# First and third GEMM by Strassen's seven products, with first result and activations kept in fp32 and split where they are used

## The chip, the cores and the metric

The kernel runs on one core of one Trainium2 chip. The metric is the device time of one execution in microseconds (us), and less is better. Five engines work side by side, each through its own list of instructions in the order in which the program writes them, and meet only at semaphores: PE (TensorE, the matmuls), DVE (VectorE), ACT (ScalarE), POOL (GpSimd) and SP, which here only issues the DMAs.

## The reference, cut to what matters

```
x = attn(q, k, v, cap)            # 2 batches, 12 heads, 448 tokens, head size 64; scores go through cap*tanh(s/cap)
x = x as 896 tokens x 768
h = x @ w_in                      # 768 x 2048, the first GEMM
g = max(0.01 * h, h)
y = g @ w_out                     # 2048 x 768, the second GEMM
yn = y / sqrt(mean(y*y) + 1e-6) * rms_g
gate = yn @ w_gate                # 768 x 1536 each: together the third GEMM
val  = yn @ w_val
out = (gate * sigmoid(gate) * val) @ w_out2     # 1536 x 768, the fourth GEMM
```

All is fp32. The matmuls run on fp32r operands: each fp32 operand is split into a rounded part (`hi`) and what is left (`lo = x - hi`), and a product is made of three matmuls, `w_hi*x_hi`, `w_hi*x_lo` and `w_lo*x_hi`.

## The kernel before

All arrays are held transposed, features on the 128 partitions and tokens on the free axis, 448 tokens of one batch to a tile. Five stages follow each other on PE.

**Attention** goes through 12 pairs of heads. For each pair PE makes scores (L611, L615) and weighs the values (L629, L633); ACT does tanh and exp (L348, L354). DVE splits q and k (`split_qk`, L432, L434), takes the result out of PSUM (`keep_x`, L442), inverts the sums that came back through a DMA (L448, L452), multiplies (`normalise`, L459) and splits the pair's x tile (L462 for `x_hi`, L464 for `x_lo`). PE cannot weigh the next pair before `keep_x` of the last one.

**First GEMM** (`unit_in`, L647): 32 units, one for each of 16 feature tiles and each batch, of 6 contraction tiles times 3 matmuls. DVE makes `w_hi` (L472), POOL `w_lo` (L296), both double buffered. The result goes through `leak` on ACT (L360), `g_full` on DVE (L478), `g_hi` on ACT (L365) and `g_lo` on DVE (L483), so that all of g lies split in SBUF when it is used.

**Second GEMM** (`unit_out`, L673): 6 output tiles of two halves, 48 matmuls each, and both batches in turn on each weight tile. ACT squares (L386), POOL sums the squares (L309), DVE scales by `rms_g` (L535), ACT and DVE split the result (L390, L541). The work behind one output tile lies beside the matmuls of the next.

**Third GEMM** (`unit_gv`, L693): 24 units of 36 matmuls, a gate and a value unit for each of 12 tiles. The sum of squares (L703) and the spread of the reciprocal root (L711) sit between the first three units. DVE multiplies (L566, L569, L572, L579), ACT does the sigmoid (L406) and `act_hi` (L410), POOL `act_lo` (L321). The fourth GEMM's weights are split during the stage (L584 on DVE, L327 on POOL).

**Fourth GEMM** (L736): 14 groups of 36 matmuls with 384 columns; ACT takes them out (L424) and SP stores them.

The order on each engine is written by hand; no scheduler moves anything. SP issues the loads in the order in which they are used, each waiting for its buffer.

## Time and profile before

| what | value |
|---|---|
| median of 3 runs | 620.59 us (620.0 to 622.28) |
| the profiled execution's own time | 620.48 us |
| its span, first to last instruction | 618.7 us |
| DVE, ACT, POOL busy | 282.0, 161.3, 203.5 us |

The span is what the rows below cut up; 1.78 us of the execution's time lie outside it. Busy time of PE counts matmuls that overlap each other in the pipeline, so the step from one matmul to the next is read from the length of a stretch over its count of matmuls. A stall of PE is a gap between such stretches.

### The profile page before, as it was taken

Reading aid. Unit: us, or ns where it says so; the run is one execution under the profiler, and the core shown is the slowest. Engines: PE = TensorE matmul, PEld = TensorE weight load, DVE = VectorE, ACT = ScalarE, POOL = GpSimd, SP = SyncE. Lnnn points to the kernel's source line nnn. Section 1 sums busy time; section 2 is a strip of 40 time slices with the busy share of each in tenths; the row PEclk is TensorE's granted clock in tenths of the full one; section 3 lists DMA queues with packets and bytes.
Section 4 is the critical chain, followed back from the end, with each engine's and each line's share of the span. In section 5 each row is a group of like instructions: output and inputs, shape, how many; then the busy total and the mean of one; then the engine's idle time right before and its main releaser. Section 6 shows DMA issues by size and latency. Waiting matters only on the chain.

```text
span 618.7 us, 7411 instructions
## 1 busy us (share of the span) xinstructions
PE 601.8 (97%) x2988; PEld 527.3 (85%) x2988; DVE 282.0 (46%) x383; ACT 161.3 (26%) x227; POOL 203.5 (33%) x124
## 2 busy tenths in 40 slices
PE   4999999989999999999999999999999999999998
PEld 3556554779999999999999999999999999999997
DVE  3286664688788883332133226344545443110000
ACT  5777775122333220111011222111111111100000
POOL 1020000245455553343353425453545352332000
PEclk9999999999999999999999999999999999999999
DMA  6145542243333332121211211212212220123101
GB/s 208 33 108 125 124 125 46 77 131 105 105 120 107 102 120 91 46 69 34 69 39 47 77 52 51 77 52 77 70 58 77 57 71 2 51 59 121 38 26 38
DMA packets 31586, 47.75 MB, mean 77 GB/s; under 512 B 17216, under 2 KB 19008, under 8 KB 31552
## 3 DMA queue, kind: packets, MB, share of 16 engines
q1 hardware_dynamic: 31552, 47.29, 26.1%
q8 instruction: 23, 0.38, 0.2%
q14 instruction: 11, 0.09, 0.1%
...
## 4 chain that ended last, share of the span: by engine, by line
PE 90%; DVE 4%; DMA 2%; POOL 1%; ACT 1%; issue 1%; SPq 0%; DVEq 0%
PE ps L693 28%; PE ps L673 19%; PE ps L647 17%; PE ps L736 13%; PE ps L629 7%; PE ps L611 2%; PE ps L633 2%; DMA qk_raw<-in_qk 1%; PE ps L615 1%; DVE x_norm L459 1%; DMA sums<-x_raw 1%; DVE g_lo L483 1%; POOL w_lo L296 1%; DVE x_raw L442 1%; ACT probs L354 1%
## 5 line engine op out<-in xcount | busy, mean ns | idle before, releaser
L296 POOL TENSOR_TENSOR w_lo<-w_raw,w_hi 128x768 fp32r<-128x768 f32 (+1 forms) x68 | 132.6, 1950 | 323.8 <-DVE w_hi L472 323.8
L472 DVE CAST w_hi<-w_raw 128x768 fp32r<-128x768 f32 (+1 forms) x68 | 39.5, 582 | 187.5 <-issue 119.8
L693 PE MATMUL ps<-x_hi,w_hi 128*128 128x448 f32 x288 | 82.0, 366 | 0.0
L693 PE MATMUL ps<-x_lo,w_hi 128*128 128x448 f32 x288 | 81.8, 365 | 0.0
L693 PE MATMUL ps<-x_hi,w_lo 128*128 128x448 f32 x288 | 81.8, 365 | 0.0
L647 PE MATMUL ps<-x_hi,w_hi 128*128 128x448 f32 x192 | 70.5, 367 | 2.9 <-POOL w_lo L296 2.9
L647 PE MATMUL ps<-x_hi,w_lo 128*128 128x448 f32 x192 | 70.1, 365 | 0.0
L647 PE MATMUL ps<-x_lo,w_hi 128*128 128x448 f32 x192 | 70.1, 365 | 0.0
L483 DVE TENSOR_TENSOR g_lo<-g_full,g_hi 128x448 fp32r<-128x448 f32 x32 | 61.0, 1910 | 0.0
L629 PE MATMUL ps<-probs,v_ones 128*128 128x448 f32 x144 | 56.2, 540 | 2.1 <-DVE x_raw L442 2.1
L693 PEld LDWEIGHTS ps<-x_hi,w_lo 128*128 128x128 f32 x288 | 54.1, 188 | 4.3
L693 PEld LDWEIGHTS ps<-x_lo,w_hi 128*128 128x128 f32 x288 | 54.1, 188 | 4.3
L693 PEld LDWEIGHTS ps<-x_hi,w_hi 128*128 128x128 f32 x288 | 53.9, 188 | 4.3
L673 PE MATMUL ps<-g_lo,w_hi 128*128 128x448 f32 x192 | 54.7, 366 | 0.0
L673 PE MATMUL ps<-g_hi,w_lo 128*128 128x448 f32 x192 | 54.7, 366 | 0.0
L673 PE MATMUL ps<-g_hi,w_hi 128*128 128x448 f32 x192 | 54.7, 366 | 0.0
L629 PEld LDWEIGHTS ps<-probs,v_ones 128*128 128x128 f32 x144 | 27.1, 190 | 25.8 <-issue 25.4
L647 PEld LDWEIGHTS ps<-x_hi,w_hi 128*128 128x128 f32 x192 | 36.1, 188 | 7.5 <-POOL w_lo L296 4.1
L348 ACT ACTIVATE probs<-ps 128x896 f32<-128x896 f32 (+1 forms) x48 | 36.8, 816 | 21.6 <-PE ps L611 21.6
L673 PEld LDWEIGHTS ps<-g_hi,w_lo 128*128 128x128 f32 x192 | 36.1, 188 | 3.1
L673 PEld LDWEIGHTS ps<-g_hi,w_hi 128*128 128x128 f32 x192 | 36.0, 188 | 3.1
L673 PEld LDWEIGHTS ps<-g_lo,w_hi 128*128 128x128 f32 x192 | 36.1, 188 | 3.1
...
## 6 DMA issues: line engine op xcount, KB each, us to landing
w_raw<-in_w_in SPq DMA_DIRECT2D x32, 384.0 KB, 3.0
...
w_raw<-in_w_gate SPq DMA_DIRECT2D x12, 384.0 KB, 2.9
w_raw<-in_w_val SPq DMA_DIRECT2D x12, 384.0 KB, 3.0
v_raw<-in_w_out SPq DMA_DIRECT2D x12, 384.0 KB, 3.0
...
```

Of the source, the lines that this page charges most:

```text
L296: pool.tensor_tensor(w_lo[u % 2][:, 0:n], w_raw[u % 2][:, 0:n], w_hi[u % 2][:, 0:n].bitcast(F32), ALU.subtract).then_inc(w_lo_done, 1)
L348: act.activation(tiles(probs_of(p, i, n), S), ps[:, bank_of(p, i):bank_of(p, i) + n, 0:S], ACT.Tanh, scale=scale_reg).then_inc(tanh_done, 1)
L354: act.activation(c, c, ACT.Exp, scale=cap_reg, bias=capc[:, 6:7]).then_inc(exp_done, 1)
L472: dve.tensor_copy(w_hi[u % 2][:, 0:n], w_raw[u % 2][:, 0:n]).then_inc(w_hi_done, 1)
L483: dve.tensor_tensor(lo[:, cols(u % N1)], g_full[u % 2][:, :], hi[:, cols(u % N1)].bitcast(F32), ALU.subtract).then_inc(g_lo_done, 1)
L611: last = pe.matmul(ps[:, bank + h, 0:S], k[HEAD[h], k_c], q[HEAD[h], 0:S], start=(k is hi and q is hi), stop=(k is lo))
L629: pe.matmul(ps[:, PV + h, 0:S], v_ones[p % 2][:, c:c + 128], probs[p % 2][:, (2 * t + h) * S:(2 * t + h + 1) * S], start=(t == 0), stop=False)
L633: last = pe.matmul(ps[:, PV + h, 0:S], v_ones[p % 2][HEAD[h], c:c + 128], probs[p % 2][HEAD[h], 2 * MAIN * S:(2 * MAIN + 1) * S], start=Fa ...
L647: last = pe.matmul(ps[:, HP + u % 2, 0:S], w[u % 2][:, c * 128:(c + 1) * 128], x[:, (b * KD + c) * S:(b * KD + c + 1) * S], start=(c == 0 ...
L673: last = pe.matmul(ps[:, 2 * (m % 2) + b, 0:S], w[half][:, (f % HALF_F) * 128:(f % HALF_F + 1) * 128], g_parts[b][g][:, f * S:(f + 1) * S] ...
L693: last = pe.matmul(ps[:, 4 * fp + 2 * s + b, 0:S], w[s][:, c * 128:(c + 1) * 128], x[:, (b * KD + c) * S:(b * KD + c + 1) * S], start=(c = ...
L736: last = pe.matmul(ps[:, n % 8, 0:NHALF], a[:, c], w[half][:, f * NHALF:(f + 1) * NHALF], start=(f == 0 and a is act_hi and w is v2_hi), s ...
```

## The change

Strassen's scheme (in Winograd's form) multiplies two matrices cut in 2 by 2 blocks with seven block products in place of eight. Here the blocks are the two halves of the contraction (3 tiles of 128 each), two feature tiles (in the third GEMM the gate tile and the value tile) and the two batches. A unit, `s`, is seven products of 9 matmuls (`product`): 8 units are the first GEMM, 12 the third. Each product has its own combination of x blocks (B11, T1, T3, T2, B22, B21, T4) and of weight blocks.

- x combinations are made once, before each of the two GEMMs: 21 tiles are split in place of 12. `combine` makes them in the attention (DVE makes T1 to T4 and all `x_hi`, POOL all `x_lo`); `first_half`, `second_half`, `t2_t3`, `t4`, `y_hi`, `y_lo`, `y_lower` make them in the second GEMM and behind it (DVE, ACT and POOL).
- Weight combinations are made for each unit: four `s_part` on DVE, 384 wide. `w_hi` is moved from DVE to ACT (`weight_hi`), `w_lo` stays on POOL (`weight_lo`), now 384 wide (256 in the second GEMM), in a ring of seven instead of two.
- Results are put together from PSUM on DVE: `take_p5`, `take_p7`, `take_p6`, and four more additions for each unit. P3, P2 and P4 add into banks that hold an earlier product, so PE waits there for `a_done`, `p1_kept` and `a2_done`.
- g stays in fp32. `g_hi` (ACT) and `g_lo` (DVE) split two tiles for each of the 48 steps of the second GEMM, into a ring of two steps; the second GEMM is now 3 passes over all of g, two output tiles by two batches each (`unit_out`, 12 matmuls for a step).
- The activations stay in fp32 as well and are split for each of the 7 token tiles of the fourth GEMM (`split_act` on ACT, `split_lower` on DVE). Its weights are split in the last gate and value unit (`value_hi` on ACT, `value_lo` on DVE, L490 on POOL), four raw buffers deep.
- silu is one activation; the second factor of the norm is put into the output's scale, where L572 was a multiplication.

The core of the diff:

```diff
-            def unit_in(u):
-
-                b = u // N1
-                pe.wait_ge(w_lo_done, u + 1)
-                if u < 2:
-                    pe.wait_ge(tanh_done, T * PAIRS)
-                at_least(pe, g_done, u - 1)
-                pe.wait_ge(x_lo_done, (b + 1) * NP)
-                for c in range(KD):
...
+            def product(s, j, c_tiles=range(KH)):
+                n = widx(s, j)
+                if c_tiles[0] == 0:
+                    pe.wait_ge(w_lo_done, n + 1)
+                    bank_free(s, j)
+                for c in c_tiles:
+                    x_ready(s, j, c)
+                    w_c = slice(n % 7 * HALF + c * 128, n % 7 * HALF + (c + 1) * 128)
                     for w, x in ((w_hi, x_hi), (w_hi, x_lo), (w_lo, x_hi)):
...
+            def unit_out(i):
+
+                q, f = divmod(i, N1)
+                n = W_OUT + i
+                pe.wait_ge(w_lo_done, n + 1)
+                pe.wait_ge(g_lo_done, 2 * i + 2)
...
+            def g_hi(i):
+
+                f = i % N1
+                if i < N1:
+                    act.wait_ge(g_done, 4 * (f // 2 + 1))
+                if i > 1:
+                    act.wait_ge(prod_done, count[W_OUT + i - 2])
+                for b in range(B):
+                    act.activation(ring_hi[:, cols(2 * (i % 2) + b)], g_tile(2 * f + b), ACT.Copy).then_inc(g_hi_done, 1)
...
+            for i in range(STEPS):
+                q, f = divmod(i, N1)
+                weight_lo(W_OUT + 5 + i)
+                if q > 0 and f in (3, 7):
+                    m = 2 * (q - 1) + (f == 7)
+                    add_squares(m, 0)
+                    add_squares(m, 1)
+                if q > 0 and f in (4, 8):
+                    m = 2 * (q - 1) + (f == 8)
+                    if m < KH:
+                        y_lo(B11, m)
+                    else:
+                        y_lo(B22, 0)
+                        y_lo(B21, 0)
...
+            s = U1
+            pe.wait_ge(sq_done, 2 * (KD - 2))
+            pe.wait_ge(scaled_done, 2 * (KD - 2))
+            product(s, P1)
+            product(s, P5)
+            pe.wait_ge(sq_done, 2 * (KD - 2) + 1)
+            pe.wait_ge(scaled_done, 2 * (KD - 2) + 2)
+            product(s + 1, P1)
+            pe.wait_ge(sq_done, 2 * KD - 1)
+            pe.wait_ge(scaled_done, 2 * KD)
+            product(s + 1, P5)
             pe.wait_ge(acc_done, 2 * KD)
...
+            for c in range(KH):
+                for j in (P7, P6, P3, P2):
+                    product(s, j, range(c, c + 1))
+                if c == 1:
+                    pe.wait_ge(rinv_done, 1)
...
+            keep_p1(UNITS - 1)
+            for k in range(7):
+                value_hi(k)
+            silu(UNITS - 1, 1)
+            value_hi(7)
+            value_hi(8)
+            value_hi(9)
+            silu(UNITS - 1, 0)
+            split_act(0, *pieces_of(0)[0])
```

Three places show how the instructions stand. First DVE in the attention, one pair's turn near the end (`r_bc` holds the pair's normalised x, `sq_67` and `sq_68` its T1 and T2; line numbers are those of each kernel's own file). Before:

```order
L448 SCALAR_TENSOR_TENSOR sums_eps<-sums_61 128x7
L452 RECIPROCAL recip_64<-sums_eps 128x7
L459 TENSOR_TENSOR x_norm<-x_raw_86,recip_row_88 64x448 x2
L462 CAST x_hi<-x_norm 128x448
L464 TENSOR_TENSOR x_lo<-x_norm,x_hi 128x448
L442 COPY x_raw_86<-ps 65x896
```

Now, for pairs 6 to 8:

```order
L711 RECIPROCAL recip_76<-sums_eps 128x7
L719 TENSOR_TENSOR r_bc<-x_raw_93,recip_row_95 64x448 x2
L742 TENSOR_TENSOR sq_67<-u_0_62,r_bc 128x448
L743 TENSOR_TENSOR sq_68<-x_hi,r_bc 128x448
L724 CAST x_hi<-r_bc 128x448
L724 CAST x_hi<-sq_67 128x448
L750 TENSOR_TENSOR sq_68<-x_lo,sq_68 128x448
L724 CAST x_hi<-sq_68 128x448
L701 COPY x_raw_93<-ps 65x896
```

Two instructions between the multiplication and `keep_x` became six, and the `x_lo` halves stand on POOL.

Second, POOL in the second GEMM. Before, two weight halves and two sums of squares for each output tile:

```order
L296 TENSOR_TENSOR w_lo_55<-w_raw_51,w_hi_53 128x1024
L296 TENSOR_TENSOR w_lo_56<-w_raw_52,w_hi_54 128x1024
L309 TENSOR_TENSOR sq_acc_94<-sq_acc_94,sq_92 128x448
L309 TENSOR_TENSOR sq_acc_95<-sq_acc_95,sq_93 128x448
L296 TENSOR_TENSOR w_lo_55<-w_raw_51,w_hi_53 128x1024
```

Now, in its third pass (one `w_lo` of 256 columns for each step of PE):

```order
L428 TENSOR_TENSOR w_lo<-w_raw_53,w_hi 128x256
L441 TENSOR_TENSOR sq_acc<-sq_acc,sq_67 128x448
L441 TENSOR_TENSOR sq_acc<-sq_acc,sq_68 128x448
L428 TENSOR_TENSOR w_lo<-w_raw_53,w_hi 128x256
L445 TENSOR_TENSOR x_lo<-p_0_58,x_hi 128x448
L445 TENSOR_TENSOR x_lo<-p_1_59,x_hi 128x448
L428 TENSOR_TENSOR w_lo<-w_raw_54,w_hi 128x256 x2
```

The x halves of the third GEMM joined the sums of squares, in the steps right behind them.

Third, DVE in the last gate and value unit and behind it. Before:

```order
L566 TENSOR_TENSOR leak_67<-ps,r_bc 128x448
L566 TENSOR_TENSOR leak_68<-ps,r_bc 128x448
L569 TENSOR_TENSOR leak_67<-leak_67,g_full_69 128x448
L569 TENSOR_TENSOR leak_68<-leak_68,g_full_70 128x448
L572 TENSOR_TENSOR leak_67<-leak_67,r_bc 128x448
L572 TENSOR_TENSOR leak_68<-leak_68,r_bc 128x448
L579 TENSOR_TENSOR a_full_103<-ps,leak_67 128x448
L579 TENSOR_TENSOR a_full_104<-ps,leak_68 128x448
```

Now (`v_lo` is the low half of the fourth GEMM's weights, `split_lo` that of the activations):

```order
L1013 TENSOR_TENSOR a_t_61<-ps,a_t_61 128x448
L1042 TENSOR_TENSOR v_lo<-w_raw_52,v_hi 128x768
L1042 TENSOR_TENSOR v_lo<-w_raw_54,v_hi 128x768
L1018 TENSOR_TENSOR sq_68<-ps,u_1_63 128x448
L1020 TENSOR_TENSOR sq_68<-sq_68,r_bc 128x448
L1042 TENSOR_TENSOR v_lo<-w_raw_52,v_hi 128x768
L1024 TENSOR_TENSOR sq_67<-ps,r_bc 128x448
L1042 TENSOR_TENSOR v_lo<-w_raw_54,v_hi 128x768
L1028 TENSOR_TENSOR u_1_63<-ps,u_1_63 128x448
L1035 TENSOR_TENSOR act_full<-a_t_61,sq_68 128x448
L1038 TENSOR_TENSOR act_full<-u_1_63,sq_67 128x448
L1049 TENSOR_TENSOR split_lo<-act_full,split_hi 128x1280
```

Four halves of the fourth GEMM's weights, and the split of ten activation tiles, came between the last products and the fourth GEMM's first matmul.

## Rows read from the trace of the kernel before

**Rows 1.** The page's first part: busy us, share of the span, instructions.
```profile
PE 601.8 (97%) x2988; PEld 527.3 (85%) x2988; DVE 282.0 (46%) x383; ACT 161.3 (26%) x227; POOL 203.5 (33%) x124
```

**Rows 2.** The chain that ended last: start us, us, engine and line.
```profile
111.28 3.86 PE ps L647 x18
...
136.84 95.12 PE ps L647 x468
231.96 117.51 PE ps L673 x576
...
366.55 160.53 PE ps L693 x792
...
532.70 83.15 PE ps L736 x474
```

**Rows 3.** Engines by stretch: length, PE, PEld, DVE, ACT, POOL busy, clock, DMA.
```profile
232.00:349.00 117.00, 117.00 (x575) 107.73 (x574) 33.81 (x36) 11.82 (x22) 43.27 (x22) 1.00 0.18 56
366.00:527.00 161.00, 161.00 (x799) 149.23 (x798) 76.49 (x120) 27.66 (x48) 74.36 (x48) 1.00 0.20 59
```

**Rows 4.** Groups by line and shape: count | busy us, mean ns | idle before.
```profile
L296 POOL TENSOR_TENSOR w_lo<-w_raw,w_hi 128x768 fp32r<-128x768 f32 x56 | 103.7, 1852 | 258.7 <-DVE w_hi L472 258.7
L483 DVE TENSOR_TENSOR g_lo<-g_full,g_hi 128x448 fp32r<-128x448 f32 x32 | 61.0, 1910 | 0.0
L296 POOL TENSOR_TENSOR w_lo<-w_raw,w_hi 128x1024 fp32r<-128x1024 f32 x12 | 28.9, 2406 | 65.1 <-DVE w_hi L472 65.1
L478 DVE TENSOR_TENSOR g_full<-ps,leak 128x448 f32<-128x448 f32 x32 | 19.9, 622 | 0.0
L365 ACT ACTIVATE g_hi<-g_full 128x448 fp32r<-128x448 f32 x32 | 18.5, 579 | 30.5 <-DVE g_full L478 30.5
L354 ACT ACTIVATE probs<-probs,capc 128x1344 f32<-128x1344 f32 x12 | 17.0, 1416 | 0.4
L464 DVE TENSOR_TENSOR x_lo<-x_norm,x_hi 128x448 fp32r<-128x448 f32 x12 | 7.5, 626 | 0.4
L462 DVE CAST x_hi<-x_norm 128x448 fp32r<-128x448 f32 x12 | 4.7, 394 | 0.4
```

**Rows 5.** DVE in order of time: start us, us, instruction.
```profile
141.92 1.90 DVE L483 TENSOR_TENSOR g_lo<-g_full,g_hi 128x448 fp32r<-128x448 f32 x1
...
273.15 3.23 DVE L541 TENSOR_TENSOR x_lo<-y_full,x_hi 128x448 fp32r<-128x448 f32 x2
```

**Rows 6.** POOL in order of time, the same two moments.
```profile
141.49 1.85 POOL L296 TENSOR_TENSOR w_lo<-w_raw,w_hi 128x768 fp32r<-128x768 f32 x1 [1.83 <-DVE w_hi L472]
...
271.99 2.41 POOL L296 TENSOR_TENSOR w_lo<-w_raw,w_hi 128x1024 fp32r<-128x1024 f32 x1 [7.38 <-DVE w_hi L472]
274.36 3.04 POOL L309 TENSOR_TENSOR sq_acc<-sq_acc,sq 128x448 f32<-128x448 f32 x2
```

**Rows 7.** DVE in one pair's turn of the attention.
```profile
96.26 1.09 DVE L442 COPY x_raw<-ps 65x896 f32<-65x896 f32 x1 [2.11 <-PE ps L633]
...
99.77 1.23 DVE L459 TENSOR_TENSOR x_norm<-x_raw,recip_row 64x448 f32<-64x448 f32 x2
...
104.35 1.09 DVE L442 COPY x_raw<-ps 65x896 f32<-65x896 f32 x1 [2.26 <-PE ps L633]
```

**Rows 8.** PE in order of time: the first matmuls, and after a stall.
```profile
7.00 0.74 PE L611 MATMUL ps<-qk_hi 64*128 64x448 f32 x2 [7.00 <-DVE qk_lo L434]
...
11.19 0.57 PE L615 MATMUL ps<-qk_lo,qk_hi 128*128 128x448 f32 x1
11.56 0.45 PE L615 MATMUL ps<-qk_hi,qk_lo 128*128 128x448 f32 x1
...
128.82 0.47 PE L647 MATMUL ps<-x_hi,w_hi 128*128 128x448 f32 x1 [2.21 <-POOL w_lo L296]
...
129.33 0.36 PE L647 MATMUL ps<-x_hi,w_lo 128*128 128x448 f32 x1
```

**Rows 9.** DMA issues: engine, count, KB each, us to landing.
```profile
w_raw<-in_w_gate SPq DMA_DIRECT2D x12, 384.0 KB, 2.9
```

1099 lines of the change are left out of this document (766 added, 333 removed).

## The prediction

> **What bounds the kernel now.** I read busy time first [rows 1]: PE is busy 97% of the span, DVE 46%, POOL 33%, ACT 26%. Then the chain of waits [rows 2]: from 136.84 us on it is four long stretches of matmuls, 95 us of the first GEMM, 118 of the second, 161 of the third, 83 of the fourth, nearly without gaps. So fewer matmuls are worth their full step, as long as what feeds them stays hidden. The step: 160.53 us for 792 matmuls of the third GEMM is 0.203 us; 117.51 for 576 of the second is 0.204; 83.15 for 474 of the fourth, with 384 columns, is 0.175. The only sizeable idle time is at the start of the first GEMM: 111.28 to 231.96 us is 120.7 where 576 steps are 116.8, so 3.9 us.
>
> Then I asked how much cover is left beside the matmuls [rows 3]. In the second GEMM's 117 us DVE works 34 and POOL 43; in the third's 161, DVE 76 and POOL 74. Those numbers hide a collision [rows 4]: `g_lo` on DVE, two SBUF inputs, takes 1910 ns, while `x_lo` of the same shape and kind, in the attention where POOL rests, takes 626. [Rows 5, 6] show why: POOL's `w_lo` runs from 141.49 to 143.34; DVE's `g_lo` starts at 141.92 and ends at 143.82, 0.48 after POOL. At 273.15 two such DVE instructions meet POOL: `w_lo` ends at 274.40, DVE's first follows, then POOL's first sum, then DVE's second at 276.38, and POOL's last ends at 277.40. They take turns, whole instruction by whole instruction: DVE holds what they share 0.47 us for 448 columns, POOL 1.02. Instructions of DVE with one input in PSUM (622 ns) do not wait. The Trainium skill (SBUF — State Buffer, "Who interferes with whom") says that two SBUF inputs on DVE and a GpSimd read exclude each other for the whole instruction; the trace agrees.
>
> **The change part by part.** Durations are from [rows 4]. POOL: 768 columns 1.85, 1024 2.41, so 2.16 ns a column: 1.02 for 384, 0.74 for 256. DVE, two SBUF inputs: 0.63 for 448, 0.56 for 384, 0.96 for 768. ACT: 0.58 for 448; from there to 1344 columns in 1.42 is 0.93 ns a column, so 0.52, 0.40 and 0.87 for 384, 256 and 768.
>
> *Matmuls.* First GEMM 8 units of 63 are 504 for 576; third 12 of 63 are 756 for 864. 180 matmuls less, at 0.203: **-36.5**. The second and fourth keep 576 and 504.
>
> *Attention.* One DVE turn [rows 7]: `keep_x` at 96.26, multiplication from 99.77 to 101.00, next `keep_x` at 104.35, 8.09 later, set by PE. So 4.74 us go to the end of the multiplication, and 3.35 are left. For pairs 6 to 8 there now follow three two-input instructions and three casts, 3 x 0.54 + 3 x 0.39 = 2.8, and two POOL `x_lo` of 1.02 fall between them: 4.8. The turn becomes 9.5. PE forgives the first 1.5 (scores stand between), then loses some 1.3 in each of two turns. Against that goes a stall of 1.2 at about 41 us, where DVE split weights in the middle of the attention. Net **+1.3** (-1.5 to +6).
>
> *Start of the first GEMM.* DVE owes the last two pairs' combinations, four `s_part` and the hidden tiles of unit 0 before `take_p5` of unit 1, for which P3 waits. I get 3.6 us of stall; before 3.9. **0** (-1 to +3).
>
> *Within units.* A unit is 63 x 0.203 = 12.8 us. DVE has 8 two-input instructions of 0.5 to 0.6 in the first GEMM (7 in the third) and 6 or 7 with PSUM at 0.54 to 0.6: about 8 us. POOL has 7 x 1.02 = 7.1; ACT some 5.3. Both sides of the shared port together hold it 10.5 of 12.8 us. The nearest deadline is `take_p5`, due when P3 starts, 7.3 us into the unit. With leftovers of the unit before and three turns given to POOL I find it done at 6.5 in the first GEMM and 7.0 in the third. **0** (0 to +10); if this cover goes, each unit pays the excess.
>
> *First to second GEMM.* The old order had all g split. Now after P4 of unit 7 come, on DVE, an addition 0.62, the leaky 0.63, the memset of 0.9, and two `g_lo` of which one waits for a 256-wide `w_lo`: 3.8 us till PE may start. **+3.8** (2.5 to 5).
>
> *Within the second GEMM.* A step is 12 x 0.204 = 2.45 us. `g_hi` may start when the step two back is complete, 2.25 before it is due, and needs 1.13 on ACT, then 0.62 on DVE: margin 0.4. In the first pass POOL's `w_lo` falls clear of `g_lo`. In the second and third pass POOL gets two sums of squares in one step and one or two `x_lo` in the next, four times. Each `g_lo` then takes its turn behind 1.02 of POOL: I lay out 1.0 lost in the step behind the sums, 1.2 in the next, 0.1 later, three times 2.3; the fourth time DVE also has `t2_t3` and POOL two `x_lo`, 4.0. Sum **+10.5** (3 to 16): nil is excluded by the margin of 0.4 against 1.02, and the low end lets half of the meetings miss.
>
> *Second to third GEMM.* PE can do P1 and P5 of unit 8 (3.65). Then `w_lo` of P1 of unit 9 ends only at 7.05, since ACT takes four squares and P1 first: stall 3.4. `w_lo` of P5 ends at 11.4, behind two more sums taking turns with `t2_t3`: 2.6. Then 15 two-input instructions on DVE, alternating with POOL's four `x_lo`, stand before the reciprocal root at 22.1, for which PE waits after c = 1 from 19.5: 2.6; restarts 0.3. Before, none of it was on the path. **+8.9** (6 to 13).
>
> *Third to fourth GEMM.* The last unit's 12.8 us do not cover its list. DVE is free for `value_lo(1)` at 8.7 and ends it at 9.6; only then can the buffer be loaded again, 3.0 with issue [rows 9], so `value_hi(5)` starts at 12.7, `value_hi(7)` at 15.3, `value_hi(9)` at 17.5, and behind it in ACT's queue silu until 18.9, `split_act` of 1280 columns until 20.2, and on DVE `split_lower`, 1.5: 21.8. PE, free at 12.8, waits 9.0; before it lost 0.4 there (527.08 to 532.70 holds 30 steps of 0.175). **+8.6** (6 to 11).
>
> *Clock.* PE's first matmul starts at 7.00 us; from 11.19 to 11.56 its steps still take 0.37 us [rows 8], where 0.203 is the rule later. So the array ran at its lower level, 1.2 GHz, though the profile's column of the granted clock prints full speed there: 4.6 us of work, of which about half is lost, 2.3. Behind the 9 us stall I take +2.0 for a like restart (0 to 2.3), and for the shorter ones nothing: after a stall of 2.21 us at 128.82 the third matmul starts 0.51 later, where two slow steps are 0.74. **+2.0**.
>
> Sum: -36.5 + 1.3 + 0 + 0 + 3.8 + 10.5 + 8.9 + 8.6 + 2.0 = -1.4. From the profiled execution's 620.48: **619.1 us**; the median of the three runs is 0.11 higher, which I leave out.
>
> **The rivals.** *The gain shows (B).* Forecast's stalls exist but the lock meetings in the second GEMM mostly miss and the two late handovers cost 6 each: 3 + 6 + 6 + 3.8 + 1.5 = 20 for 34, so 605 to 611. For it: the layout of two dozen hand-placed turns errs both ways, and POOL has five steps of slack, so its order can slip. Against: strict turns in [rows 5, 6], and ACT's chain of buffers, which meets no lock.
>
> *DVE becomes the bound within the units (C), slower.* `take_p5` misses P3's start. In the third GEMM the margin is 0.3 us. One more turn behind POOL (1.0) in each of ten units of the third, and half as much in six of the first, gives +13 us: 632. It decides as soon as DVE's chain from P4's end to `take_p5` exceeds 7.3 us. For it: eight turns against 7.1 us of POOL; against: POOL's arrivals are spread by PE's own products, and a PE that stalls gives the turn back.
>
> *The clock falls (D), slower.* If also the stalls of 2.6 to 3.8 us put the array at the lower level, as in [rows 8], four more restarts of up to 2.3 make +7 to +9: 627. The row behind the stall of 2.21 us speaks against it, and no row shows one of 3.8. The Trainium skill (TensorE: Matmul & The Clock Gate, "What's actually happening") says that the throttled clock is the default and activity releases it; the first 4.6 us agree, and no stretch of this trace shows a fall after work had begun.
>
> That the change does not do what it says is excluded by the count of matmuls: 180 less.
>
> **How the numbers follow.** Forecast 0.52, B 0.28, C 0.12, D 0.08. The forecast's own range is 612 to 627, from its bounds (the larger ones taken with their squares: 7, 4, 3 and 4). About half a per cent, 3.1 us, is what a measurement of this kernel can tell from no change. The forecast's 0.52 divides into 0.15 faster, 0.22 same, 0.15 slower; B is faster, C and D slower except 0.01. Faster 0.42, same 0.23, slower 0.35. For 8 in 10 I take 604 to 632.
>
> **What would show each step.** Right: PE's busy matmuls near 2800 records; gaps before the first step of the second GEMM (3 to 4 us), between the products of units 8 and 9 (three of 2.5 to 3.5) and before the fourth GEMM (about 9); `g_lo` with a mean between 0.6 and 1.0 us and single ones over 1.5 behind `sq_acc`; and waits for `p1_kept` or `a_done` inside the units near zero. Wrong: a second GEMM of under 122 us (collisions too dear), a unit of over 13.3 us (C), matmul spacing of 0.37 behind a short stall (D), or a gap before the fourth GEMM under 6, which would mean that ACT's chain of buffers runs faster than DVE's place in the list allows.

## The result: 16.6 us slower

| what | before | after |
|---|---|---|
| median | 620.5 us | 637.1 us (636.13 to 640.94) |
| the profiled execution's own time | 620.48 us | 637.12 us |
| its span | 618.7 us | 635.3 us |

The ratio is 1.0274, interval 1.0227 to 1.032. The forecast was 619.1 us and its range ended at 632. From here on, times "from A to B us" are in the profiled execution of the kernel named.

The first part of the page of after, and two rows of its second part, in 40 equal slices (the second is the granted clock):

```profile
PE 582.0 (92%) x2805; PEld 501.2 (79%) x2805; DVE 419.2 (66%) x567; ACT 278.3 (44%) x475; POOL 274.0 (43%) x244
...
PE   4998988789999979998988969899999995899998
...
PEclk9999999899999989999998979999999999899999
```

Against [rows 1], PE has 183 records less and 19.8 us less busy, where 180 steps of 0.203 would be 36.5. Its share fell from 97 to 92%, so idle time came in. And the clock row has 8 and 7 in it, where the mean clock of before was 1.000; of after it is 0.979. Where PE waited, from the trace's waits of after (engine and line, what ended the wait: us in total, times, longest):

```profile
PE ps L1118 <- DVE x_raw L701: 9.3, 4, 3.5
PE ps L1258 <- DVE split_lo L1049: 9.0, 1, 9.0
PE ps L1213 <- DVE ring_lo L906: 7.8, 10, 1.8
...
PE ps L1167 <- issue: 4.5, 3, 2.1
PE ps L1167 <- POOL w_lo L428: 4.0, 2, 3.7
PE ps L1213 <- POOL w_lo L428: 3.9, 1, 3.9
PE ps L1104 <- ACT probs L500: 2.4, 2, 1.2
...
PE ps L1167 <- DVE a_t L799: 1.6, 1, 1.6
```

Read as a map of the stages: L1118 is the attention (before, PE waited 2.1 us in all for L442 there), L1167 the first and third GEMM, L1213 the second, L1258 the fourth. The row with `issue` holds three waits whose cause the profile does not name; by their places in the program the longest (2.1 us, at 140.75) is for `take_p5` of unit 1, one is at the third GEMM's entry, and one, of 1.18 us, is for `take_p7` of unit 9. So two waits lie inside the units of the third GEMM, this one and the 1.6 us for `a_t` in unit 10. DVE's rows in front of them, then PE's:

```profile
400.53 0.61 DVE L805 TENSOR_TENSOR a_t<-ps,a_t 128x448 f32<-128x448 f32 x1
...
408.86 1.37 DVE L783 TENSOR_TENSOR s_sum<-s_sum,w_raw 128x384 f32<-128x384 f32 x1
...
411.44 0.61 DVE L799 TENSOR_TENSOR a_t<-ps,p 128x448 f32<-128x448 f32 x1
```

```profile
401.25 0.44 PE L1167 MATMUL ps<-x_hi,w_hi 128*128 128x448 f32 x1 [1.18 <-issue]
...
412.19 0.44 PE L1167 MATMUL ps<-x_hi,w_hi 128*128 128x448 f32 x1 [1.60 <-DVE a_t L799]
```

The chain that ended last, its longest pieces (start us, us, engine and line), beside [rows 2]:

```profile
148.37 80.94 PE ps L1167 x396
233.19 48.61 PE ps L1213 x228
...
412.19 115.16 PE ps L1167 x567
541.77 90.56 PE ps L1258 x504
```

The long stretches still run at the old step: 80.94 / 396 is 0.204 us, 115.16 / 567 is 0.203. Outside units 9 and 10 the unit of 63 matmuls costs what was forecast; what was lost lies between such pieces.

**The clock.** The granted clock and PE's work in short stretches of after (stretch: length, busy us of PE, of PE's weight loads (PEld), DVE, ACT and POOL with their counts, clock, DMA share, GB/s):

```profile
142.00:144.00 2.00, 2.00 (x7) 1.81 (x6) 1.90 (x5) 0.00 (x0) 0.00 (x0) 0.50 0.00 0
234.00:236.50 2.50, 2.50 (x9) 2.22 (x8) 0.69 (x2) 0.00 (x0) 0.00 (x0) 0.50 0.24 93
340.00:342.00 2.00, 2.00 (x7) 1.74 (x7) 2.00 (x3) 0.00 (x0) 2.00 (x3) 0.50 0.00 0
374.00:379.00 5.00, 3.76 (x11) 2.87 (x10) 4.43 (x5) 1.40 (x4) 5.00 (x4) 0.50 0.02 5
543.00:544.00 1.00, 1.00 (x5) 1.00 (x4) 1.00 (x3) 0.34 (x1) 0.32 (x1) 0.50 0.00 0
```

In each the clock is 0.50, the lower level of 1.2 GHz. The first of them matmul by matmul (PE in order of time: start us, us, instruction):

```profile
138.31 0.37 PE L1167 MATMUL ps<-x_hi,w_lo 128*128 128x448 f32 x1
140.75 0.44 PE L1167 MATMUL ps<-x_hi,w_hi 128*128 128x448 f32 x1 [2.08 <-issue]
...
141.64 0.42 PE L1167 MATMUL ps<-x_lo,w_hi 128*128 128x448 f32 x1
141.85 0.58 PE L1167 MATMUL ps<-x_hi,w_lo 128*128 128x448 f32 x1
142.23 0.58 PE L1167 MATMUL ps<-x_hi,w_hi 128*128 128x448 f32 x1
...
145.21 0.38 PE L1167 MATMUL ps<-x_hi,w_lo 128*128 128x448 f32 x1
145.44 0.37 PE L1167 MATMUL ps<-x_hi,w_hi 128*128 128x448 f32 x1
```

A stall of 2.24 us beyond the step (138.31 to 140.75), five steps of 0.2, then nine of 0.37 (141.85 to 145.21 is 3.36), then 0.2 again: 9 x 0.17 = 1.5 us lost. In [rows 8] a stall of nearly the same length, 2.21 us, cost nothing of the kind. Outside the attention after has five such places: behind the stalls at 138.31, 228.92, 337.26, 368.61 and 532.44. The excess of their steps over 0.2035 us (0.175 in the fourth GEMM), summed from the trace, is 1.7, 1.7, 1.7, some 2.5 and 1.3 us; with 1.5 in the attention (the 12 matmuls from 114.82 on take 6.29 us, those of the turn before 4.75) it is some 10 us.

**The ledger.** Each stage is taken from the start of its first matmul to the start of its last, each gap from there to the next stage's first, one step of 0.2 us included. Only between the second and the third GEMM, where nothing stalls, the boundary is set at the last matmul but one of the second, in every kernel. "Forecast" is before plus the terms of the prediction. These are the stage lengths of all sections below.

| stage | before | forecast | after | miss | of it clock |
|---|---|---|---|---|---|
| to the end of the attention | 111.2 | 112.5 | 122.0 | +9.5 | 1.5 |
| first GEMM | 120.4 | 105.8 | 106.9 | +1.1 | 1.7 |
| first to second GEMM | 0.2 | 4.0 | 4.3 | +0.3 | |
| second GEMM | 117.1 | 127.6 | 131.6 | +4.0 | 3.4 |
| third GEMM | 177.8 | 164.8 | 167.7 | +2.9 | 2.5 |
| third to fourth GEMM | 0.2 | 8.8 | 9.3 | +0.5 | |
| fourth GEMM | 88.6 | 90.6 | 90.2 | -0.4 | -0.7 |

The misses add up to 17.9 of 18.0 us (637.12 - 619.1); behind the fourth GEMM 3.2 us were left before and 3.4 after.

One trace is one execution. Seven traces have this attention unchanged (after, and c1, h1, g1, g2, s1 and t1 below), and in them it ended at 118.0 to 122.0 us. So 121.99 is the upper end of what this code does, and a difference between two traces in a stage that no edit touches means nothing.

### The profile page after: what moved, and what is told of

It reads as the page before. It is cut to its first block, busy times and chain, and to the rows that moved or that the text cites. A ratio compares the mean times of both kernels' runs of the same rounds, so it can differ in the third digit from the quotient of the medians.

```text
span 635.3 us, 7890 instructions
## 1 busy us (share of the span) xinstructions
PE 582.0 (92%) x2805; PEld 501.2 (79%) x2805; DVE 419.2 (66%) x567; ACT 278.3 (44%) x475; POOL 274.0 (43%) x244
## 4 chain that ended last, share of the span: by engine, by line
PE 64%; DVE 12%; issue 3%; ACT 1%; DMA 1%; POOL 0%; DVEq 0%; ACTq 0%
PE ps L1167 34%; PE ps L1213 14%; PE ps L1258 14%; DVE ring_lo L906 4%; DVE x_lo L955 1%; DMA w_raw<-in_w_out 1%; PE ps L1118 1%; ACT ring_hi L543 1%; DVE s_sum L777 1%; DVE s_sum L783 1%; DVE g L949 0%; DVE g L938 0%; DVE g L914 0%; DVE g L940 0%; ACT w_hi L523 0%
## 5 line engine op out<-in xcount | busy, mean ns | idle before, releaser
L428 POOL TENSOR_TENSOR w_lo<-w_raw,w_hi 128x384 fp32r<-128x384 f32 (+1 forms) x108 | 115.4, 1071 | 146.5 <-ACT w_hi L523 141.2
L1167 PE MATMUL ps<-x_hi,w_hi 128*128 128x448 f32 x420 | 156.0, 371 | 10.1 <-issue 4.5
L1167 PE MATMUL ps<-x_hi,w_lo 128*128 128x448 f32 x420 | 155.2, 369 | 0.0
L1167 PE MATMUL ps<-x_lo,w_hi 128*128 128x448 f32 x420 | 155.1, 369 | 0.0
L428 POOL TENSOR_TENSOR w_lo<-s_sum,w_hi 128x384 fp32r<-128x384 f32 x80 | 88.9, 1119 | 65.6 <-ACT w_hi L523 65.5
L906 DVE TENSOR_TENSOR ring_lo<-g,ring_hi 128x448 fp32r<-128x448 f32 x96 | 68.3, 755 | 45.9 <-ACT ring_hi L543 45.0
L1167 PEld LDWEIGHTS ps<-x_hi,w_hi 128*128 128x128 f32 x420 | 79.8, 190 | 19.6 <-issue 12.7
L1167 PEld LDWEIGHTS ps<-x_hi,w_lo 128*128 128x128 f32 x420 | 80.0, 190 | 6.4
L1167 PEld LDWEIGHTS ps<-x_lo,w_hi 128*128 128x128 f32 x420 | 80.0, 191 | 6.2
L543 ACT ACTIVATE ring_hi<-g 128x448 fp32r<-128x448 f32 x96 | 50.2, 570 | 53.3 <-PE ps L1213 53.3
L1213 PE MATMUL ps<-ring_hi,w_hi 128*128 128x448 f32 x192 | 57.0, 379 | 11.7 <-DVE ring_lo L906 7.8
L1118 PE MATMUL ps<-probs,v_ones 128*128 128x448 f32 x144 | 58.0, 553 | 9.3 <-DVE x_raw L701 9.3
L1213 PE MATMUL ps<-ring_lo,w_hi 128*128 128x448 f32 x192 | 56.3, 375 | 0.0
L1213 PE MATMUL ps<-ring_hi,w_lo 128*128 128x448 f32 x192 | 56.3, 375 | 0.0
L523 ACT ACTIVATE w_hi<-w_raw 128x384 fp32r<-128x384 f32 (+1 forms) x108 | 50.2, 466 | 13.1 <-PE ps L1167 11.3
L1118 PEld LDWEIGHTS ps<-probs,v_ones 128*128 128x128 f32 x144 | 27.6, 195 | 34.7 <-issue 32.1
L1258 PE MATMUL ps<-v_hi,split_hi 128*128 128x384 f32 x168 | 46.2, 345 | 9.0 <-DVE split_lo L1049 9.0
L1213 PEld LDWEIGHTS ps<-ring_hi,w_hi 128*128 128x128 f32 x192 | 35.8, 192 | 19.4 <-POOL w_lo L428 8.1
L1258 PE MATMUL ps<-v_lo,split_hi 128*128 128x384 f32 x168 | 45.8, 342 | 0.0
L1258 PE MATMUL ps<-v_hi,split_lo 128*128 128x384 f32 x168 | 45.7, 342 | 0.0
```

Of the source, the lines that this page charges most:

```text
L428: pool.tensor_tensor(w_lo[:, c], source, w_hi[:, c].bitcast(F32), ALU.subtract).then_inc(w_lo_done, 1)
L523: act.activation(w_hi[:, c], w_source(n), ACT.Copy).then_inc(w_hi_done, 1)
L543: act.activation(ring_hi[:, cols(2 * (i % 2) + b)], g_tile(2 * f + b), ACT.Copy).then_inc(g_hi_done, 1)
L906: dve.tensor_tensor(ring_lo[:, c], g_tile(2 * f + b), ring_hi[:, c].bitcast(F32), ALU.subtract).then_inc(g_lo_done, 1)
L1118: pe.matmul(ps[:, PV + h, 0:S], v_ones[p % 2][:, c:c + 128], probs[p % 2][:, (2 * t + h) * S:(2 * t + h + 1) * S], start=(t == 0), stop=False)
L1167: last = pe.matmul(ps[:, base(s) + BANK_OF[j], 0:S], w[:, w_c], x[:, xs(j, c)], start=(j in (P1, P5, P7, P6) and c == 0 and w is w_hi and ...
```

## The experiments

All are edits of the changed kernel unless the text says otherwise. The kernel before measured 619.98 to 620.9 beside them. Mechanism W: the waits of PE cost their own length. Mechanism C: the clock behind them costs extra. Mechanism Q: the attention is late through the order of a queue.

**c1_warm: fill the stalls with matmuls.** Idle products into unused banks, 17 ahead of the second GEMM, 15 between the products of units 8 and 9, 46 ahead of the fourth:

```
+            fill(0, x_hi[:, 0:128], x_hi[:, cols(0)], S, 17)
             for i in range(STEPS):
                 unit_out(i)
```

> Three blocks of filler matmuls whose results are overwritten unread (17 before the second GEMM, 15 between the products of units 8 and 9, 46 with 384 columns before the fourth GEMM) sit where the changed kernel's TensorE stalls 4.1, 3.9 and 9.1 us. They change nothing else. Theory 1 (the stalls themselves cost about what was laid out, and what comes on top is the clock, which falls to 1.2 GHz after them): the stretches of 0.37 us steps behind these three places vanish, worth 1.7 + 3.4 + about 1.5 to 3, so the kernel is 6 to 8 us faster than the changed one, 629 to 631 us, with a granted clock above 0.99. Rival (the fillers only lengthen the queue, the slow steps come from the new stage's own operands or are tied to stage starts): steps behind the stalls stay at 0.37 and the time stays at 637 or rises by a us or two. The stall behind unit 1's fifth product and the one in the third pass are not filled, so two low stretches of 3.4 us should remain in any case, and the one in the attention.

Measured: 631.98 us (631.75 to 634.9), ratio 1.0201 (1.0157 to 1.0245), so 5.1 less, under the 6 to 8 expected. The low clock at 234 and 543 us was gone; the fourth GEMM took 87.3 us for 90.2, and the second 130.0 for 131.6. Behind the third GEMM's entry a longer stretch at 1.2 GHz stood in spite of the fill (third GEMM 169.7 for 167.7). So C is real at two of three places, worth some 1.5 us each. Of the 2.9 us of the fourth GEMM only 1.4 are slow steps: its other steps take 0.1733 us here and 0.1767 in after, and they take 0.1733 in g1_no_sums too, where nothing is filled; why is open. And of the 5.1 us the attention (120.6 for 122.0) and the first GEMM (105.7 for 106.9, with no 1.2 GHz behind its stall of 2.2 us) gave some 2.6 without any fill.

**a1_order: the queue of SP.** In after, the load of `w_in` (384 KB) is issued ahead of the small DMA that spreads the sums, on which DVE's reciprocal waits.

```
-                if p < 4:
-                    load_raw(p, w_in[p])
                 spread_sums(p)
+                if p < 4:
+                    load_raw(p, w_in[p])
```

> In the attention the first four loads of the first GEMM's weights are issued behind the small DMA of the sums instead of ahead of it; nothing else moves. Theory 1 (that load delays the sums, 5.6 us from keep_x to landing where it was 3.2, and sets DVE back 2.5 us by the fourth pair, and the lateness then meets the late qk loads): sums land 3.2 to 3.7 us after keep_x in pairs 0 to 3, attention ends 2 to 3 us earlier, 634 to 635 us. Rival (the 2.7 us of s_part in the fourth turn and the three-combination turns are all of it): attention ends within 0.7 us of where it did, 636.5 to 637.5 us.

Measured: 630.48 us (629.45 to 632.95), ratio 1.0169 (1.0125 to 1.0214); the attention ended at 114.5 for 122.0, far more than expected. DVE in the fourth turn, of after and then of this kernel:

```profile
38.58 1.09 DVE L701 COPY x_raw<-ps 65x896 f32<-65x896 f32 x1 [0.97 <-PE ps L1122]
41.67 0.66 DVE L691 CAST qk_hi<-qk_raw 128x960 fp32r<-128x960 f32 x1 [2.01 <-DMA qk_raw<-in_qk]
...
46.09 0.17 DVE L707 SCALAR_TENSOR_TENSOR sums_eps<-sums 128x7 f32<-128x7 f32 x1 [2.56 <-DMA sums<-x_raw]
```

```profile
38.51 1.09 DVE L701 COPY x_raw<-ps 65x896 f32<-65x896 f32 x1 [3.23 <-PE ps L1122]
39.52 0.65 DVE L691 CAST qk_hi<-qk_raw 128x960 fp32r<-128x960 f32 x1
...
41.90 0.17 DVE L707 SCALAR_TENSOR_TENSOR sums_eps<-sums 128x7 f32<-128x7 f32 x1 [0.54 <-DMA sums<-x_raw]
```

From `keep_x` to the sums 7.5 us against 3.4, and DVE's idle time ends on two DMAs instead of on PE. SP issues in the order of its list: a late reciprocal makes its store late (36.50 us in after, 34.18 here), and right behind that store stands the next `qk` load (36.93, 34.61). One late turn is handed on to the next, and so a cause of 4 us in one turn can cost more than 4 at the end. The next `keep_x` starts at 46.60 us here, and at 49.2 to 50.4 in the seven traces with the old order. Against their ends of the attention, 118.0 to 122.0, the edit is worth 3.5 to 7.5 us, and by the medians of all runs 6.6. Q holds.

**a3_xlo_late: also POOL's low parts behind all of a pair's casts.**

```
-                    pool.wait_ge(x_hi_done, x_count[part])
+                    pool.wait_ge(x_hi_done, x_before(p + 1))
```

> The load order of a1_order, and in the attention POOL starts a pair's low halves only when DVE has written all of the pair's high halves, so that DVE is not made to take turns within its combination. Theory 1 (two turns of 1.02 us behind POOL stretch the turns of pairs 6 to 8 over the 8.1 us of PE): DVE's second cast of those turns takes 0.4 us instead of 1.1 and the late addition 0.6 instead of 1.6, the two stalls of 2.0 and 2.2 us that a1_order has left in the attention go, and with them a low clock stretch of 3.4 us: attention ends at 111.5 to 112.5 us, 2 to 4 us faster than a1_order, 626.5 to 628.5 us. Rival (the three more DVE instructions alone fill the turn): stalls stay over 1 us each, 629.5 us or more.

Measured: the attention ended at 111.2 us, as before the change (the same in m1, m2 and m3 below, which have this edit). In after, DVE's turn of pair 6 shows what went:

```profile
91.28 1.58 DVE L750 TENSOR_TENSOR sq_acc<-x_lo,sq_acc 128x448 f32<-128x448 f32 x1
93.00 1.10 DVE L724 CAST x_hi<-sq_acc 128x448 fp32r<-128x448 f32 x1
94.02 1.08 DVE L701 COPY x_raw<-ps 65x896 f32<-65x896 f32 x1
```

The addition takes 1.58 and even the cast 1.10 us, where the same two take 0.62 and 0.40 in this kernel, with POOL at rest. But the time was 629.99 us (628.04 to 631.06), ratio 1.0148 (1.0118 to 1.0177), hardly under a1_order and over the 626.5 to 628.5 expected: 3.3 us were won in the attention, and the third GEMM took 169.3 us, 1.6 more than in after, with 1.2 GHz on two stretches. The low clock comes and goes from run to run.

**h1_split_early: the first piece of the fourth GEMM's input split ahead of the last `v2` pieces**, on ACT and DVE alike:

```
             keep_p1(UNITS - 1)
+            split_act(0, *pieces_of(0)[0])
             for k in range(7):
                 value_hi(k)
...
```

> The first token tile's split of ten activation tiles (their activations are complete one unit earlier) is moved in front of the last unit's weight splits on ACT, and in front of take_p7 on DVE; nothing else moves. Theory 1 (the 9.1 us before the fourth GEMM are this split's place behind the weight splits, whose buffers wait for DMAs): the gap falls to under 1 us, 1 to 4 us come back as waits for the fourth GEMM's last weight tiles (f = 9 to 11), and the low clock behind the gap goes too: 7 to 10 us faster, 627 to 630 us. Rival (the weight splits are late by themselves, PE only changes what it waits for): 3 us or less, 634 us or more.

Measured: 630.4 us (624.6 to 631.45), ratio 1.0133 (1.0069 to 1.0197). The gap of 9.3 us went to 0.2, a new stall of 2.5 us stands one piece later, at 543 us. So the 9 us were the order of a list and not the load of the engines, as the prediction had laid it out; of 9.3 us, 6.7 came through by the medians.

**g1_no_sums and g2_spread: the port in the second GEMM.** The first leaves POOL's eight sums of squares out of it. The second keeps them, one in a step instead of two, with the `x_lo` halves in the steps behind:

```
-                if q > 0 and f in (3, 7):
-                    m = 2 * (q - 1) + (f == 7)
-                    add_squares(m, 0)
-                    add_squares(m, 1)
+                if q > 0 and f in (3, 4, 7, 8):
+                    add_squares(2 * (q - 1) + (f > 4), f in (4, 8))
...
```

> Leaves out the eight POOL additions that sum the squares within the second GEMM's second and third pass (the norm is then wrong); semaphores are still raised, all else is as in the changed kernel. Theory 1 (each DVE split of g takes its turn behind one POOL instruction of 1.02 us, and PE has 0.4 us of margin): of the 11 us that the second GEMM loses beside the clock some 5 to 7 go, and one low clock stretch (1.7) with them if the largest stall falls under 2 us; 629 to 633 us. Rival (DVE's own extra work, first_half, t2_t3, y_lower, is what delays g_lo): under 2.5 us, 634.5 us or more.

> The same 13 extra POOL instructions of the second GEMM's second and third pass, but one in a step (sums in steps 3, 4, 7, 8, low halves in 5, 9, 10) instead of two in one step and one or two in the next. Theory 1 (one instruction of 1.02 us fits nearly between two splits of g, two do not): the stalls of 0.9 and 1.1 us behind them shrink to about 0.5 in sum each time, second GEMM 127 to 129 us instead of 131.6; 632 to 635 us. Rival (any such instruction costs its 1.02 us less the margin of 0.4 wherever it stands, so 13 x 0.6): no shorter, 636 to 638 us.

Measured: 630.92 us (629.85 to 634.22), ratio 1.0186 (1.0139 to 1.0232), second GEMM 126.7 for 131.6; and 632.43 us (628.24 to 636.83), ratio 1.021 (1.0162 to 1.0259), second GEMM 128.7. The meeting in after, DVE and then POOL:

```profile
326.13 2.40 DVE L906 TENSOR_TENSOR ring_lo<-g,ring_hi 128x448 fp32r<-128x448 f32 x2 [1.30 <-ACT ring_hi L543]
328.45 1.16 DVE L955 TENSOR_TENSOR x_lo<-a_t,x_hi 128x448 fp32r<-128x448 f32 x1
329.53 2.66 DVE L906 TENSOR_TENSOR ring_lo<-g,ring_hi 128x448 fp32r<-128x448 f32 x2
...
325.39 2.66 POOL L441 TENSOR_TENSOR sq_acc<-sq_acc,sq 128x448 f32<-128x448 f32 x2
328.01 1.11 POOL L428 TENSOR_TENSOR w_lo<-w_raw,w_hi 128x256 fp32r<-128x256 f32 x1
329.09 1.53 POOL L445 TENSOR_TENSOR x_lo<-extra,x_hi 128x448 fp32r<-128x448 f32 x1
```

Each `ring_lo` takes 1.2 or 1.3 us instead of 0.63 as long as POOL has something queued. But the stage lengths mix two things. The stalls of the stage, summed from the trace as the excess of the steps over 0.2035 us with the clock's stretches left out, are 9.6 us in after, 6.5 without the sums (single ones of 0.84 and 1.05) and 8.2 with the sums spread (single ones of 1.11 and 1.98). In both variants the second of after's two stretches at 1.2 GHz was missing, 1.6 us. Without the sums the stall in front of it had shrunk from 1.99 to 0.85 us; with the sums spread it still stood, 1.98 us, and no fall came, which is chance, as k3 and k4 below show. So the sums are worth 3.1 us of the 9.6 and one fall, and spreading them 1.4. Of the expected 5 to 7 us that is half. What the rest is, POOL's `x_lo` halves or DVE's own added work, was not taken apart.

**s1_g2start: the first g tile ahead of the last hidden tiles.** The gap between first and second GEMM in after, on DVE:

```profile
229.33 0.62 DVE L831 TENSOR_TENSOR g<-ps,u 128x448 f32<-128x448 f32 x1 [0.62 <-PE ps L1167]
229.99 0.62 DVE L836 SCALAR_TENSOR_TENSOR g<-g 128x448 f32<-128x448 f32 x1
230.75 0.81 DVE L899 MEMSET sq_acc<- 128x896 f32 x1
231.47 3.22 DVE L906 TENSOR_TENSOR ring_lo<-g,ring_hi 128x448 fp32r<-128x448 f32 x4
```

```
+            g_lo(0)
+            hidden_11(U1 - 1)
+            hidden_21(U1 - 1)
             for i in range(STEPS):
                 q, f = divmod(i, N1)
-                g_lo(i)
+                if i:
+                    g_lo(i)
+                if i == 3:
...
+                    dve.memset(sq_acc[:, :], 0.0).then_inc(squares_zeroed, 1)
```

> The changed kernel with one edit: the high and low part of the second GEMM's first g tile are made ahead of the last two hidden tiles on ScalarE and VectorE, and the zeroing of the sum of squares comes three steps later. If the 4.1 us that TensorE waits between the first and second GEMM come from the queue of VectorE in front of g_lo(0), the wait falls below 1 us. If the low clock of 233 to 237 us is set off by that wait, it goes with it, and the second GEMM loses another 1.6 us: together about 5 us, ratio 1.018 to 1.022 against the kernel before. If the low clock comes by itself at this place, it stays, and only 3 to 4 us are gained.

Measured: 631.2 us (630.34 to 632.23), ratio 1.0189 (1.0172 to 1.0206): 5.9 less. The gap fell from 4.3 to 0.2 us and no 1.2 GHz followed; the second GEMM took 130.7 for 131.6. In the profiled execution the two stages that the edit touches are worth 4.1 + 0.9 = 5.0 us, W and most of C together; 5.9 is the difference of the medians.

**t1_handover and m1_mended: entry into the third GEMM.** The first takes the weight sums of unit 9 ahead of the last squares on ACT and POOL; the second has this and the mends of a3, h1 and g2, takes the reciprocal root earlier, and has the further moves that its expectation lists.

```
             squares(KD - 2)
-            squares(KD - 1)
-            keep_p1(U1)
             weight_hi(widx(U1 + 1, P1))
+            squares(KD - 1, (0,))
+            weight_hi(widx(U1 + 1, P5))
+            squares(KD - 1, (1,))
+            keep_p1(U1)
...
```

> Between second and third GEMM ACT and POOL split the two weight blocks of unit 9 that PE needs next ahead of the sums of squares. Theory 1 (each stall there is the place of one weight split in two queues): the stalls of 3.9 and 1.6 us become under 1.5 in sum; the wait for the reciprocal root, which was 0.7, grows by some 2 to 4 us, since DVE's list behind it is no shorter; the low clock of 6.8 us shrinks to 3.4. Net 0 to 3 us faster, 634 to 637 us. Rival (PE's stalls there are only the clock's): the whole sum goes, 5 us and more, 632 us or less.

> All edits that take away a named wait: loads of w_in 0 and 1 at the start and s_part of unit 0 in the second turn, the low halves of the attention behind the high ones, take_p5 of unit 1 ahead of the last pair, the spread sums, t1_handover with the reciprocal root ahead of three s_part and its transposes one contraction tile later, and the early split of h1. Theory 1 (the change's matmul gain of 36.5 us is whole and only waits and the clock ate it): attention ends at 112 us (-10), first GEMM 104 (-3), second 128 (-4), entry to the third -3, entry to the fourth -8: 607 to 612 us, faster than both kernels. Rival (each wait removed is replaced by the next one behind it, as DVE and POOL together hold the port most of the time): 618 us or more.

Measured: 637.75 us (635.88 to 641.17), ratio 1.0285 (1.0243 to 1.0326), and 620.61 us (616.56 to 622.97), ratio 0.999 (0.9966 to 1.0013). Both missed, m1 its 607 to 612 by 8.6 us. In t1 the stall of 3.86 us fell to 1.67 and 1.21, but the one for the root grew to 2.86 and the third GEMM took 170.8 us for 167.7. The squares lie on a path of their own, over the root to the scaling, and are as urgent as the weights.

**m2_mended: all mends without that hand-over, with s1's.** As in m1_mended, two of the four loads of `w_in` are issued ahead of the first pair and two in turns 8 and 9, and the four `s_part` of unit 0 come in turn 1 instead of 3.

> All mends together on the changed kernel: the w_in loads behind the sums' DMA, the low part of x on GpSimd behind all high parts, the sums of the second GEMM spread, the fourth GEMM's inputs split early, and the first g tile split ahead of the last hidden tiles; the last GEMM's hand-over as in the changed kernel. From the mended kernel with the other hand-over (620.6 us): third GEMM entry -1 to -2, start of the second GEMM -4 with its low clock -1.6, so 612 to 615 us, ratio 0.985 to 0.992: a little faster than the kernel before. If the low clock moves to another stall instead of going, 616 to 619 us, ratio 0.993 to 0.998. If the product of the saved matmuls is eaten by something else than these waits, it stays at 620.

Measured: 612.94 us (611.27 to 614.26), ratio to the kernel before 0.9891 (0.9872 to 0.9909): 7 us faster than before, 24.2 faster than after. The single mends, each against 637.1, were a3 -7.1, h1 -6.7, g2 -4.7 and s1 -5.9: -24.4. They add up, as edits in different stages would, though each difference has in it the few us by which executions of one kernel differ (g2 alone 628.24 to 636.83). Its stages: attention 111.2, first GEMM 108.4, gap 0.2, second 129.4, third 167.7, gap 0.2, fourth 89.2.

**m3_entry: one instruction of the hand-over alone**, the high part of the ninth unit's first sum ahead of the last two squares.

> The mended kernel (612.9 us) with one instruction of ScalarE moved: the high part of the ninth unit's first weight sum stands ahead of the last two squares instead of behind them. The squares wait for GpSimd's sums (L443), and TensorE waits 3.9 us for the low part of that weight (L430). Expected: the wait falls to about 2.3 us, and in some runs the low clock behind it goes: -1.5 to -3 us, 610 to 611.5 us. Rival: the squares' sums come later and the wait for the root behind product 8 grows by as much: no change, 613 us.

Measured: 615.35 us (612.67 to 619.08), ratio 0.9926 (0.99 to 0.9952), no gain on m2_mended. The stall of 3.86 us became 2.43 and 2.38 and the third GEMM 168.7 us for 167.7. The rival's result, though not its place: the root's wait was gone, and the time was lost one stall earlier.

**k1_stalls, k2_filled, k3_rising, k4_falling: the clock by itself.** These are the kernel before with stalls in its third GEMM, where PE otherwise never rests: ACT makes copies, each waiting for the last, and PE waits for the last one. k2_filled has idle matmuls ahead of each wait.

```
...
+                    for k in range(PLAN[f][0]):
+                        done = sum(PLAN[j][0] for j in PLAN if j < f) + k
+                        if done:
+                            act.wait_ge(stall_done, done)
+                        act.activation(ident[:, 64:128], ident[:, 0:64], ACT.Copy).then_inc(stall_done, 1)
...
+                    pe.wait_ge(stall_done, sum(PLAN[j][0] for j in PLAN if j <= f))
```

> The kernel before, with four stalls of TensorE put into its third GEMM behind hidden tiles 3, 5, 7 and 9: 5, 8, 13 and 30 copies on ScalarE, each waiting for the last, which TensorE waits for, about 1.7, 2.7, 4.5 and 10 us. Everything else is as before and the clock of the kernel before is full from its start to its end. If a stall of 2 us or more sets off a stretch at 1.2 GHz by itself, the three longer ones are each followed by about 3.4 us of matmuls at double length and the first by none. If length alone is not what decides, some of the longer ones are followed by none. Rival: the changed kernel's falls come from something else (its block products, its fp32 tiles), and no stall here lowers the clock but the 10 us one.

> As the last run, but TensorE multiplies 5, 9, 16 and 38 idle 448-column products (about 0.2 us each) into an unused bank in front of each wait, so that most of each stall is filled with work. If it is TensorE's idleness that lowers the clock, no stretch at 1.2 GHz follows and the span is some 1.7 us shorter for each stretch that is gone; if it is the stall of the other engines or the place, the stretches stay.

Measured in one run each: 643.45 and 639.9 us. The stretches behind the four stalls of k1 (1.70, 2.57, 4.00 and 8.89 us long), then behind the longest of k2, same columns as above:

```profile
411.50:414.00 2.50, 2.50 (x14) 2.33 (x13) 1.47 (x2) 0.81 (x2) 2.50 (x3) 1.00 0.10 18
443.50:446.00 2.50, 2.50 (x14) 2.27 (x13) 0.05 (x1) 0.33 (x1) 2.50 (x3) 1.00 0.49 157
478.00:481.00 3.00, 3.00 (x9) 2.66 (x9) 0.00 (x0) 0.00 (x0) 3.00 (x3) 0.50 0.00 1
519.00:522.00 3.00, 3.00 (x9) 2.66 (x9) 0.00 (x0) 0.00 (x0) 2.94 (x3) 0.50 0.00 0
```

```profile
510.00:515.00 5.00, 5.00 (x26) 4.63 (x26) 0.77 (x1) 4.46 (x18) 0.35 (x1) 1.00 0.23 79
```

14 matmuls in 2.5 us behind the short ones, 9 in 3.0 us behind the long ones. k1's third GEMM is 201.5 us, 23.7 over before: 17.2 of stalls and some 5 to 6 of slow steps. In k2 no step of that stage was slow. So at these two places it was PE's own idleness that counted, with all other engines as in k1, in one execution of each. But in the unchanged first GEMM of k2, at the place of [rows 8], a stall of 1.97 us was followed by slow steps this time:

```profile
125.24 0.37 PE L656 MATMUL ps<-x_hi,w_lo 128*128 128x448 f32 x1
127.41 0.48 PE L656 MATMUL ps<-x_hi,w_hi 128*128 128x448 f32 x1 [1.81 <-POOL w_lo L298]
...
128.37 0.57 PE L656 MATMUL ps<-x_lo,w_hi 128*128 128x448 f32 x1
128.74 0.57 PE L656 MATMUL ps<-x_hi,w_lo 128*128 128x448 f32 x1
```

So the one row on which the forecast had rested comes out either way. The kernel before shows the same by itself: of its 43 executions beside these experiments 20 have a mean granted clock of 0.997 and not 1.000, and one fall that costs 1.7 us of 618 makes 0.997. Where those falls lay no trace shows.

> The kernel before, with nine stalls of TensorE in its third GEMM, behind hidden tiles 2 to 10, made of 6 to 14 chained copies on ScalarE: by the two stalls measured so far (8 copies 2.57 us, 13 copies 4.00 us) about 2.0, 2.3, 2.6, 2.9, 3.1, 3.4, 3.7, 4.0 and 4.3 us. If length decides, the first three or four leave the clock at 2.4 GHz and all behind them are followed by 1.2 GHz: five or six falls of 3.4 or 6.8 us. If a short stall lowers it only now and then, whatever its length above 2 us, falls are scattered over the row.

> The same nine stalls in the other order, the longest first. If length decides, falls follow the first five or six stalls and none the last three; if place or what was idle before counts, the same places as in the last run show them.

Measured in one run each: 657.04 and 659.75 us. Excess of the steps behind each stall, summed from the trace:

| stall, us | 1.99 | 2.28 | 2.57 | 2.86 | 3.15 | 3.43 | 3.71 | 4.00 | 4.30 |
|---|---|---|---|---|---|---|---|---|---|
| rising: slow steps cost | 1.6 | 0 | 0 | 0 | 1.7 | 0 | 1.7 | 1.7 | 1.6 |
| falling: slow steps cost | 0 | 0 | 1.4 | 1.6 | 0 | 2.6 | 1.6 | 1.6 | 2.3 |

Neither expectation holds alone. With k1, stalls from 3.7 us up were followed by 1.2 GHz 8 times of 8, those from 2.0 to 3.4 us 5 times of 13, and not at the same lengths or places in the two runs. In the variants of the changed kernel, too, each stall of 3.8 us and more behind the attention had it (left unfilled). Of their shorter ones, 2.0 to 3.4 us, it was 23 of 34, counting after with its eleven variants. A fall costs 1.4 to 2.7 us on top of the stall.

## Why the prediction was wrong

*Matmuls, right.* The long pieces run at 0.203 to 0.204 us a step. m2_mended shows that the saving is there to be had.

*Within units (rival C), nearly right.* Nil was forecast. From the middle of unit 10 on the third GEMM runs 567 matmuls, nine units' worth, without a wait, and the first GEMM its last 396, and C's +13 us did not come. But in units 9 and 10 of the third GEMM PE waited 1.35 us for `take_p7` and 1.76 for `take_p5` (the stalls that end at 401.25 and 412.19, steps of 1.55 and 1.96 us less the 0.2 of a step), 3.1 us that the forecast had at nil. Just before, DVE's `s_part` take 1.37 us each beside POOL's `w_lo`, where the forecast counts 0.56 and the turns. It is C's mechanism, in two units instead of sixteen.

*The four hand-laid layouts, right in their sums and partly by luck.* First to second GEMM 4.1 for 3.8; the second's stalls 11.1 for 10.5 (the stage's 131.6 less 117.1 and less 3.4 of clock); second to third 9.3 for 8.9; third to fourth 9.1 for 8.6 (both gaps less that of before). The two gaps came out as laid. In the second GEMM the prediction's own terms, three times 2.3 and 4.0, make 10.9 and not 10.5, and by places it measured 2.2, 1.7, 4.0 and 1.7; leaving out the sums (g1_no_sums) took away only 3.1 us of these 9.6. At the third GEMM's entry the three stalls were laid out as 3.4, 2.6 and 2.6 and measured 3.9, 1.6 and 0.6; the sum is right because the 3.1 us of units 9 and 10 took the place of what was missing.

*Attention, the first step that failed: +1.3 forecast, +10.8 measured (+6.8 to +10.8 in the seven traces), outside its own range of +6.* The step counted what DVE does in pairs 6 to 8 and missed what is behind an instruction that moves on SP's queue. The load of `w_in` was put ahead of the sums' DMA; a1_order took 7.5 us of the 10.8 away by moving it back (6.6 by the medians). The other 3.3 went with a3_xlo_late: additions and casts of DVE, counted as 0.54 and 0.39 us, take up to 1.58 and 1.10 beside POOL. The 1.5 of clock went with the late turns. The queue of loads was followed for the fourth GEMM's buffers and not here.

*The clock, the second step that failed: +2.0 forecast, for the 9 us stall alone, some 10 us measured, at six places.* Rival D had the mechanism, "four more restarts of up to 2.3 make +7 to +9", and two of the places, the entries into the second and the third GEMM; three more falls came in the attention and behind stalls of 2.2 and 2.0 us. It was given a chance of 0.08 on one row, a stall of 2.2 us without a fall [rows 8]. One such row can't say no: of the 13 stalls from 2.0 to 3.4 us in k1, k3 and k4 8 had none either, and the forecast itself held two stalls of 3.4 and 3.8, for which no row spoke. The Trainium skill (TensorE: Matmul & The Clock Gate, "What's actually happening") has the throttled clock as the default that activity releases, and the runs agree. That 619.1 and D's 627 were both exceeded is the sum of the two steps: 619.1 + 9.5 (1.5 of it clock) + 6.9 of clock elsewhere = 635.5, and 1.6 is left for small terms. Behind the 9 us gap itself it cost 1.3 for 2.0.

*Start of the first GEMM.* Forecast 3.6 us of stall; measured 2.2 and 0.5, with 1.7 of clock: right in sum by luck.

*The range.* It was said to combine the larger bounds, 7, 4, 3 and 4, by their squares; that makes 9.5 us to either side, where 612 to 627 has 7.5. The measured time lies outside both, and outside the 604 to 632 given for 8 cases in 10.

What stays open: what decides between the short stalls that lower the clock and those that don't. Why the third GEMM loses 9 us at its entry in whatever order was tried, t1, m1 and m3, is only argued: ACT, POOL and DVE are all late by a similar amount there. What makes up the two thirds of the second GEMM's stalls that are not the sums of squares. And why the attention's length differs by 4 us between executions of the same code.
